# Attention and two MLPs in one kernel: the first eight heads' first queries unsplit, other places for the first MLP's operations, biases in two buffer sets

## The chip, the cores and the metric

The kernel runs on one core of a Trainium2 chip. The metric is the device time of one execution in microseconds (us), the median of several runs. The core has five engines that run side by side and meet at semaphores: TensorE (PE in the rows; its loads of the stationary operand are PEld), VectorE (DVE), ScalarE (ACT), GpSimd (POOL), and SyncE (SP), which issues the DMAs. "Cold" below means TensorE at 1.2 GHz, "warm" at 2.4 GHz.

## What is computed

Four batches of eight heads, 576 positions, head width 64. Per head, with a causal mask and a bias from a running sum, then a soft-max and the product with the values:

```python
scores = scale * np.matmul(q, k.transpose(0, 1, 3, 2))
cum = np.cumsum(np.maximum(s, 0.0), axis=-1)
bias = -(cum[:, :, :, None] - cum[:, :, None, :])
scores = np.where(causal, -1000000000.0, scores + np.minimum(bias, 0.0))
scores = scores - np.max(scores, axis=-1, keepdims=True)
attn = np.exp(scores)
attn = attn / (np.sum(attn, axis=-1, keepdims=True) + 1e-09)
out = np.matmul(attn, v)
```

The heads' outputs, side by side, are 2304 tokens of 512 numbers. They go through a first MLP (512 to 1024, h times its soft-max, a layer norm, 1024 to 512) and a second one (512 to 2048, h * clip(h + 3, 0, 6) / 6, 2048 to 512). All in float32.

## The kernel before

**Arithmetic.** Most products are made of split operands: a float32 tensor x is stored as hi (x rounded to the fp32r type) and lo = x - hi, and TensorE multiplies hi*hi, hi*lo and lo*hi, each in one pass of fp32r. The splits cost ScalarE a copy (hi) and VectorE or GpSimd a subtraction (lo). For q and k, ScalarE makes qk_hi (L1124), GpSimd puts q_lo into the lower half (L610) and makes k_lo (L613), so that one product over 128 rows holds two terms; a second one with k_lo (L722) follows. Probabilities are transposed on TensorE (L736), copied as hi by ScalarE (L1155), and their lo made by VectorE (L953); values are split by GpSimd (L627, L629) and multiplied in two parts (L761), whose halves ScalarE copies (L1163) and VectorE adds (L973).

**Units and items.** A unit is a pair of heads and one of two kinds of queries of it: first queries (0 to 255) or second ones (256 to 575). A batch has four units of the first kind, then four of the second. A unit of the first kind has two items (one a head, with its two tiles of 128 queries), one of the second kind five. So units 0 to 3 are items 0 to 7, units 4 to 7 items 8 to 27, and there are 112 items.

**Slots.** Every engine's program is one loop over slot numbers n, and what it does in slot n is written out by hand (L873 TensorE, L1047 VectorE, L1210 ScalarE, L668 GpSimd, L534 SyncE). In slot n TensorE transposes the probabilities of item n, multiplies the values of a unit that has ended (two slots after its last item began, SUMS_AT), and makes the scores of item n + 2. VectorE takes the bias and the row maximum of item n + 1 (L944) and then splits the probabilities of item n; ScalarE copies those of item n and takes the exponential of item n + 1 (L1132). An engine's instructions run in the order written: one that waits holds up all behind it.

**The first MLP** has 18 tiles of 128 tokens, each with six steps r = 0 to 5, spread evenly over the slots from STARTS[t] to STARTS[t + 1] (L84). Steps 0 to 2: TensorE makes the hidden values (L794), which fill two PSUM banks. Step 3: VectorE takes their maximum (max1, L1009). Step 4: ScalarE takes the exponential (exp1, L1182), VectorE the product with it (solu, L1018). Step 5: ScalarE squares (L1188, written over the hidden values in PSUM), GpSimd makes the reciprocal deviation (L648, L650). In the next tile's step 0 VectorE normalises (L1027), in steps 1 and 2 TensorE transposes (L807), ScalarE copies (L1195), VectorE splits (L1034). Steps 3 to 5 also hold the products with w_out of tile t - 2 (project, L823), whose results VectorE copies (copy_x2, L1040). TensorE may begin the hidden values of tile t + 1 once the squares of tile t are done (L782). A tile's input xs_hi and xs_lo is made by VectorE (L1004) in slot X_AT and by GpSimd (L655) one slot later; X_AT is STARTS[t] - 3, or the slot in which the last unit of these tokens is scaled, if that is later (L184 to L190). That later slot is 10 for tiles 0 and 1, 30 for tile 2, 58 for tile 6, 114 for tile 15.

In slots 3 to 10 ScalarE splits w_in (L1171) in eight parts, VectorE and GpSimd make four lo parts each; from slot 24 on w_out is split (L1176, L997); from slot 120 on GpSimd splits the first weights of the second MLP (L663, L665). SyncE issues nearly all loads in one queue. The bias of a head, its row of the running sum spread over 128 partitions, is loaded from memory into one buffer for each of two heads (L486), after the maximum of the unit that used it before; for unit 0 TensorE spreads it (L869) and ScalarE copies it (L1167).

**The second MLP** follows slot END: 96 rounds of products with 384 columns (L843 to L845) and 512 columns (L860 to L862), where TensorE is busy all the time.

## Time and profile before

| | us |
|---|---|
| median of 3 runs | 921.59 (917.24, 921.59, 922.11) |
| the profiled execution, its own time | 918.19 |
| its span, first to last instruction | 916.4 |
| TensorE busy | 845.5 (92%) |
| VectorE, ScalarE, GpSimd busy | 441.9, 412.8, 296.5 |

The busy time of TensorE is that of pipelined instructions with modelled ends, so "busy" is not "at its peak". The stretch to about 497 us holds attention and the first MLP, the rest the second MLP.

### The profile page before, as it was taken

How to read it: one execution, taken by the hardware profiler on the slowest of the kernel's cores; microseconds unless marked ns; L12 is line 12 of the kernel's file. 1: busy time of each engine (PE TensorE's matmuls, PEld its weight loads, DVE VectorE, ACT ScalarE, POOL GpSimd, SP SyncE). 2: the span in 40 equal slices, each digit the busy share in tenths (PEclk: the TensorE clock that was granted, in tenths of full speed). 3: DMA queues.
4: the chain of work that ended last, by engine and by line, in shares of the span. 5: the costliest groups of instructions: out<-in, count | busy, mean ns of one | idle time of the engine just before them, and what ended most of it. 6: DMA issues, size and time to landing. Idle time of an engine off the chain costs nothing.

```text
span 916.4 us, 13790 instructions
## 1 busy us (share of the span) xinstructions
PE 845.5 (92%) x4916; PEld 750.7 (82%) x4916; DVE 441.9 (48%) x1061; ACT 412.8 (45%) x911; POOL 296.5 (32%) x391
## 2 busy tenths in 40 slices
PE   7778779989899998999898999999999999999997
PEld 5566668888688887888787999989898999999996
DVE  3747767776676767667455232232322232332222
ACT  6745766657566566555223243232322232322222
POOL 7764466455644465453165253000000000000000
PEclk9789879999999999999999999999999999999999
DMA  7536434334434344331402040000000000000000
GB/s 232 176 111 208 119 97 141 96 99 125 124 95 115 91 115 123 108 113 40 137 2 92 1 138 1 35 1 1 35 0 1 35 1 1 35 1 1 35 1 34
DMA packets 39426, 66.84 MB, mean 73 GB/s; under 512 B 4480, under 2 KB 16512, under 8 KB 39360
## 3 DMA queue, kind: packets, MB, share of 16 engines
q1 hardware_dynamic: 39360, 65.97, 23.7%
q8 instruction: 40, 0.66, 0.3%
q14 instruction: 26, 0.21, 0.1%
HBM read 61.16 MB, written 4.79 MB: 72 GB/s over the span
## 4 chain that ended last, share of the span: by engine, by line
PE 69%; DVE 10%; ACT 9%; issue 5%; POOL 4%; DMA 2%; SPq 0%; DVEq 0%; ACTq 0%; POOLq 0%
PE psum L794 9%; PE psum L843 7%; PE psum L845 7%; PE psum L861 7%; PE psum L844 7%; PE psum L862 7%; PE psum L860 7%; PE psum L761 4%; PE psum L823 3%; PE psum L736 3%; ACT prob L1132 3%; ACT p_hi L1155 2%; DVE es L1018 2%; PE psum L807 2%; PE psum L722 2%
## 5 line engine op out<-in xcount | busy, mean ns | idle before, releaser
L1086 DVE SCALAR_TENSOR_TENSOR act<-act,psum 128x384 f32<-128x384 f32 x96 | 53.2, 554 | 286.8 <-ACT act L1240 286.8
L1240 ACT ACTIVATE act<-psum,three 128x384 f32<-128x384 f32 x96 | 55.9, 582 | 285.7 <-PE psum L845 285.7
L843 PE MATMUL psum<-x_hi,w_hi 128*128 128x384 f32 x384 | 129.5, 337 | 0.9 <-DVE x_lo L1044 0.9
L845 PE MATMUL psum<-x_hi,w_lo 128*128 128x384 f32 x384 | 129.5, 337 | 0.0
L844 PE MATMUL psum<-x_lo,w_hi 128*128 128x384 f32 x384 | 129.0, 336 | 0.0
L862 PE MATMUL psum<-w_hi,g_lo 128*128 128x512 f32 x288 | 113.9, 395 | 0.0
L861 PE MATMUL psum<-w_lo,g_hi 128*128 128x512 f32 x288 | 113.7, 395 | 0.0
L860 PE MATMUL psum<-w_hi,g_hi 128*128 128x512 f32 x288 | 112.0, 389 | 0.0
L953 DVE TENSOR_TENSOR p_lo<-psum,p_hi 128x512 fp32r<-128x512 f32 (+2 forms) x128 | 71.9, 572 | 79.5 <-ACT p_hi L1155 79.0
L1155 ACT ACTIVATE p_hi<-psum 128x512 fp32r<-128x512 f32 (+2 forms) x128 | 62.3, 500 | 96.0 <-PE psum L736 63.1
L610 POOL TENSOR_TENSOR qk_hi<-qk_raw,qk_hi 64x256 fp32r<-64x256 f32 (+1 forms) x64 | 57.0, 891 | 125.3 <-ACT qk_hi L1124 124.1
L823 PE MATMUL psum<-lnT_hi,w_out_hi 128*128 128x256 f32 x288 | 83.2, 289 | 9.9 <-DVE xT L1040 9.7
L1132 ACT ACTIVATE prob<-prob,nmax 128x128 f32<-128x128 f32 (+4 forms) x144 | 83.2, 580 | 12.2 <-DVE nmax L944 12.0
L736 PE MATMUL psum<-ident,prob 128*128 128x128 f32 x400 | 67.9, 290 | 20.7 <-ACT prob L1132 17.6
L823 PE MATMUL psum<-lnT_lo,w_out_hi 128*128 128x256 f32 x288 | 82.2, 285 | 0.0
L823 PE MATMUL psum<-lnT_hi,w_out_lo 128*128 128x256 f32 x288 | 82.2, 285 | 0.0
L736 PEld LDWEIGHTS psum<-ident,prob 128*128 128x128 f32 x400 | 49.3, 147 | 33.2 <-ACT prob L1132 28.4
L843 PEld LDWEIGHTS psum<-x_hi,w_hi 128*128 128x128 f32 x384 | 72.1, 188 | 5.3 <-DVE x_lo L1044 1.1
L844 PEld LDWEIGHTS psum<-x_lo,w_hi 128*128 128x128 f32 x384 | 72.1, 188 | 4.0
L722 PE MATMUL psum<-qk_lo,qk_hi 128*128 128x128 f32 (+2 forms) x192 | 73.8, 388 | 0.0
L794 PE MATMUL psum<-w_in_hi,xs_hi 128*128 128x512 f32 x144 | 60.9, 423 | 12.7 <-POOL xs_lo L655 12.7
L613 POOL TENSOR_TENSOR qk_lo<-qk_raw,qk_hi 128x256 fp32r<-128x256 f32 (+1 forms) x64 | 70.9, 1108 | 5.0
(95 smaller groups left out, 1881.6 us busy)
## 6 DMA issues: line engine op xcount, KB each, us to landing
qk_raw<-qk SPq DMA_DIRECT2D x32, 480.0 KB, 3.5
qk_raw<-qk SPq DMA_DIRECT2D x32, 256.0 KB, 2.7
bias<-cum_dram SPq DMA_DIRECT2D x32, 256.0 KB, 3.9
v_raw<-v_rows SPq DMA_DIRECT2D x32, 160.0 KB, 3.1
bias_tail<-cum_dram SPq DMA_DIRECT2D x32, 144.0 KB, 3.8
out<-out_sb SPq DMA_DIRECT2D x6, 768.0 KB, 3.5
w_raw<-w_in SPq DMA_DIRECT2D x16, 256.0 KB, 3.2
w_raw<-w_out SPq DMA_DIRECT2D x16, 256.0 KB, 4.1
```

The lines of the kernel that those rows point to most:

```text
L722: last = pe.matmul(ps, q, qk_lo[p][:, keys], start=False, stop=(part != 0))
L736: last = pe.transpose(dst, prob[:, src:src + P], ident[:, :])
L794: last = pe.matmul(bank(h_bank(t) + half), x, w, start=(n % 12 == 0), stop=(n % 12 == 11))
L823: last = pe.matmul(bank(L_BANK, PJW), w, x, start=(n == 0), stop=(n == 23))
L843: pe.matmul(ps, w2_hi[f][:, cols], xh, start=(c_ == 0), stop=False)
L844: pe.matmul(ps, w2_hi[f][:, cols], xl, start=False, stop=False)
L845: last = pe.matmul(ps, w2_lo[f][:, cols], xh, start=False, stop=(c_ == NC - 1))
L860: pe.matmul(bank(4 + k), gh, w2_hi[f][:, NC * P:], start=(f == 0), stop=False)
L861: pe.matmul(bank(4 + k), gh, w2_lo[f][:, NC * P:], start=False, stop=False)
L862: last = pe.matmul(bank(4 + k), gl, w2_hi[f][:, NC * P:], start=False, stop=(f == NF2 - 1))
L1132: sc.activation(p, p, ACT.Exp, scale=-1.0, bias=nmax[:, u % 2, col:col + 1], accum_out=rsum[:, u % 2, col:col + 1]).then_inc(exp_done, 1)
L1155: sc.activation(hi, ps, ACT.Copy).then_inc(pT_hi_done, 1)
```

## The change

1. **Units 0 to 3** (the first eight heads' first queries, items 0 to 7) are multiplied unsplit. q and k of a pair lie in one float32 tile of 128 partitions, one head in each half (qk_plain), and the scores are float32 products over 64 rows. The bias comes in through TensorE: a product of a one-hot column and the running sum's hi and lo rows (cum_parts) is added into the same PSUM region, and VectorE's maximum reads zeros in the bias's place. VectorE, no longer ScalarE, copies the transposed probabilities, whole; the values are float32 of both heads side by side (v_pair), one product a block; ScalarE copies the sums to their place, and VectorE adds nothing. No split by ScalarE, VectorE or GpSimd is left for these units.
2. The running sum is made first for 256 positions, and whole in VectorE's slot 0.
3. **Biases** lie in one buffer set for each kind of unit, so that a unit of one kind doesn't wait for the set of the other.
4. **Places.** STARTS; w_in is loaded from slot 2 on and split from slot 6 on (before 0 and 3); w_out is loaded in eight parts from slot 15 on (before whole, in slot 18) and split from slot 27 on (before 24).
5. **Order in a slot.** VectorE does max1 (step 3) and solu (step 5, before step 4) right behind the row maxima, ahead of the probabilities. ScalarE does exp1 and the squares behind the probabilities, exponentials and sums (before ahead of them). The squares go to a tile of SBUF, and the next tile's hidden values wait for solu, not for the squares.

```diff
-STARTS = [12, 21, 31, 37, 44, 51, 59, 65, 71, 77, 84, 90, 96, 102, 109, 115, 121, 127, 133]
+STARTS = [13, 25, 33, 39, 45, 54, 60, 66, 72, 78, 84, 90, 96, 103, 110, 116, 122, 129, 135]
-W_IN_FROM, W_OUT_FROM, EARLY_FROM = 3, 24, 120
+W_IN_LOAD = 2
+W_IN_FROM = 6
+W_OUT_LOAD = 15
+W_OUT_FROM = 27
+EARLY_FROM = 120
+PLAIN = 4
+PLAIN_ITEMS = BASE[PLAIN]
...
# SyncE: the first loads
-            load_qk(0, 0)
-            load_qk(0, 1)
-            load_qk(1, 0)
+            for u in range(PAIRS):
+                load_plain(u)
+                load_pair(u)
+            load_qk(PLAIN, 0)
             sp.wait_ge(cum_done, 1)
             sp.dma_start(cum_dram, cum[:, :]).then_inc(cum_stored, 16)
-            load_qk(1, 1)
+            load_qk(PLAIN, 1)
+            load_qk(PLAIN + 1, 0)
             sp.wait_ge(cum_stored, 16)
...
# TensorE: scores of units 0 to 3
+                    if u < PLAIN:
+                        rows = slice(0, P) if e is None else slice(e * DH, (e + 1) * DH)
+                        q = qk_plain[u][rows, q_at:q_at + P]
+                        for lo_, hi_ in [(0, w)] if w <= BANK else [(0, w // 2), (w // 2, w)]:
+                            pe.matmul(psum[:, at + lo_:at + hi_], q, qk_plain[u][rows, QW[c] + lo_:QW[c] + hi_],
+                                      start=True, stop=False)
+                            if n <= 1:
+                                pe.wait_ge(cum_parts_done, n + 1)
+                            h = head_of(u, e)
+                            last = pe.matmul(psum[:, at + lo_:at + hi_], heads[rows, h:h + 1].broadcast_to([DH, P]),
+                                             cum_parts[rows, lo_:hi_], start=False, stop=hi_ <= diag0)
+                            if hi_ > diag0:
+                                mask = mask_tail if e is None else mask_bf
+                                last = pe.matmul(psum[:, at + diag0:at + hi_], ident_bf[:, :], mask[:, 0:hi_ - diag0],
+                                                 start=False, stop=True)
+                        continue
...
# TensorE: their values
+                    if u < PLAIN:
+                        p, v_at = plain_values(u)
+                        last = pe.matmul(psum[:, o_at + q:o_at + width], v_pair[p][:, v_at + j, :, :].rearrange("p a d -> p (a d)"),
+                                         p_plain[:, src:src + width - q], start=(j == 0), stop=(j == blocks - 1))
+                        continue
...
# TensorE: hidden(t)
-                    wait(pe, sq_done, t - 1 if t >= NT - 2 else t)
+                    wait(pe, solu_done, t - 1 if t >= NT - 2 else t)
...
# TensorE: the start
-            pe.wait_ge(cum_done, 1)
-            for e in range(2):
-                pe.matmul(bank(H_BANK + e, CUT), ident[0:NH, e:e + 1].broadcast_to([NH, P]), cum[:, 0:CUT],
-                          start=True, stop=True).then_inc(bias_spread, 1)
             pe.wait_ge(mask_tail_done, 2)
-            pe.wait_ge(zeros_done, 1)
+            pe.wait_ge(heads_done, 2)
...
# VectorE: slot n
                 if 0 <= n + 1 < ITEMS:
                     for tile, e, col in TILES[n + 1]:
                         row_max(n + 1, tile, e, col)
+                if r == 3:
+                    max1(t)
+                if r == 5:
+                    solu(t)
                 if r == 0 and t >= 3:
                     copy_x2(2 * (t - 3) + 1)
-                if 0 <= n < ITEMS:
+                if 0 <= n < PLAIN_ITEMS:
+                    copy_plain(n)
+                    if n == 0:
+                        sum_all()
+                elif 0 <= n < ITEMS:
                     split_probs(n)
+                if n in SCALES_AT:
+                    scale_pair(SCALES_AT[n])
                 if r == 4 and t >= 2:
                     copy_x2(2 * (t - 2))
-                if n in SCALES_AT:
-                    scale_pair(SCALES_AT[n])
...
-                if r == 3:
-                    max1(t)
-                if r == 4:
-                    solu(t)
...
# ScalarE: slot n
-                if r == 4:
-                    exp1(t)
-                if r == 5:
-                    square(t)
-                if 0 <= n < ITEMS:
+                if PLAIN_ITEMS <= n < ITEMS:
                     copy_probs(n)
                 if 0 <= n + 1 < ITEMS:
                     for i, (tile, e, col) in enumerate(TILES[n + 1]):
                         exp_row(n + 1, i, tile, col)
                 for u, e in SUMS_AT.get(n, ()):
-                    copy_corr(u, e)
+                    if u < PLAIN:
+                        copy_sums(u, e)
+                    else:
+                        copy_corr(u, e)
+                if r == 4:
+                    exp1(t)
+                if r == 5:
+                    square(t)
...
-    nc = bacc.Bacc("TRN2", target_bir_lowering=False, num_devices=1)
+    nc = bacc.Bacc("TRN2", target_bir_lowering=False, num_devices=1, dynamic_dma_scratch_size=4096)
```

## Rows read from the trace of the kernel before

**Rows 1.** The page: busy us of each engine, its share of the span, instructions.
```profile
PE 845.5 (92%) x4916; PEld 750.7 (82%) x4916; DVE 441.9 (48%) x1061; ACT 412.8 (45%) x911; POOL 296.5 (32%) x391
```

**Rows 2.** Stretches: busy us (instructions) of PE, PEld, DVE, ACT, POOL; granted clock, DMA share, GB/s.
```profile
51.00:442.00 391.00, 350.79 (x2346) 307.01 (x2347) 265.96 (x697) 240.35 (x557) 203.06 (x283) 0.96 0.37 110
442.00:497.00 55.00, 48.17 (x305) 42.72 (x304) 30.70 (x54) 15.55 (x27) 31.13 (x36) 0.97 0.29 96
```

**Rows 3.** The waits of PE over the span: total us, times, longest.
```profile
PE psum L736 <- ACT prob L1132: 17.6, 23, 2.3
PE psum L794 <- POOL xs_lo L655: 12.7, 4, 3.8
PE psum L823 <- DVE xT L1040: 9.7, 12, 1.5
PE psum L717 <- DVE nmax L944: 5.5, 5, 2.3
```

**Rows 4.** Timeline of PE: start, us, instruction, [idle before <- releaser]; slots 0, 8, 13, and tiles 0, 2.
```profile
9.90 0.90 PE L736 MATMUL psum<-ident,prob 128*128 128x128 f32 x3 [0.30 <-ACT prob L1132]
34.19 0.84 PE L736 MATMUL psum<-ident,prob 128*128 128x128 f32 x3
51.18 0.80 PE L794 MATMUL psum<-w_in_hi,xs_hi 128*128 128x512 f32 x1 [3.77 <-POOL xs_lo L655]
55.86 0.68 PE L736 MATMUL psum<-ident,prob 128*128 128x128 f32 x3
58.16 0.39 PE L794 MATMUL psum<-w_in_lo,xs_hi 128*128 128x512 f32 x1
124.15 0.79 PE L794 MATMUL psum<-w_in_hi,xs_hi 128*128 128x512 f32 x1 [2.95 <-POOL xs_lo L655]
```

**Rows 5.** Timeline of the start: copies of unit 0's spread bias; pace of scores and values.
```profile
6.03 0.38 ACT L1167 ACTIVATE bias<-psum 128x256 f32<-128x256 f32 x1 [0.83 <-PE psum L869]
6.88 0.38 ACT L1167 ACTIVATE bias<-psum 128x256 f32<-128x256 f32 x1 [0.47 <-PE psum L869]
7.39 0.52 PE L717 MATMUL psum<-qk_hi 128*128 128x256 f32 x1
8.62 0.52 PE L717 MATMUL psum<-qk_hi 128*128 128x256 f32 x1
18.25 0.56 PE L761 MATMUL psum<-p_hi,v_sp 128*128 128x256 f32 x1
19.14 0.52 PE L761 MATMUL psum<-p_hi,v_sp 128*128 128x256 f32 x1
```

**Rows 6.** Groups by form, first 34 us: count, busy us, mean ns, idle before.
```profile
L1155 ACT ACTIVATE p_hi<-psum 128x384 fp32r<-128x384 f32 x8 | 3.9, 481 | 1.9 <-PE psum L736 1.9
L1124 ACT ACTIVATE qk_hi<-qk_raw 128x512 fp32r<-128x512 f32 x8 | 4.9, 624 | 2.3 <-DMA qk_raw<-qk 2.3
```

**Rows 7.** Timeline of POOL: the last w_in part before tile 0's xs_lo.
```profile
46.09 1.27 POOL L641 TENSOR_TENSOR w_in_lo<-w_in_raw,w_in_hi 128x512 fp32r<-128x512 f32 x1
```

**Rows 8.** Timeline: tile 10's exp1, what stood behind it, and TensorE's wait.
```profile
347.76 1.12 ACT L1182 ACTIVATE es<-psum,nmax 128x1024 f32<-128x1024 f32 x1 [1.54 <-DVE nmax L1009]
348.86 0.48 ACT L1155 ACTIVATE p_hi<-psum 128x384 fp32r<-128x384 f32 x1
350.41 0.35 PE L823 MATMUL psum<-lnT_hi,w_out_hi 128*128 128x256 f32 x1 [1.42 <-DVE xT L1040]
```

**Rows 9.** The squares and exp1, every one: duration ns min/median/max, first and last start.
```profile
L1188 ACT ACTIVATE psum<-es,neg_mu x18: 1101/1119/1122, 77.1 to 492.6; 128x1024 f32<-128x1024 f32 x18
L1182 ACT ACTIVATE es<-psum,nmax x18: 1093/1117/1120, 70.7 to 489.4; 128x1024 f32<-128x1024 f32 x18
```

**Rows 10.** ScalarE in slot 28: w_out's split.
```profile
111.55 0.71 ACT L1176 ACTIVATE w_out_hi<-w_out_raw,g_sb 128x512 fp32r<-128x512 f32 x1
```

**Rows 11.** Timeline of DVE, after attention: max1 of tiles 15 and 16.
```profile
459.96 1.22 DVE L1009 TENSOR_REDUCE nmax<-psum 128x1 f32<-128x1024 f32 x1 [0.52 <-PE psum L794]
473.21 1.23 DVE L1009 TENSOR_REDUCE nmax<-psum 128x1 f32<-128x1024 f32 x1 [0.53 <-PE psum L794]
```

More of the change, by code:

```diff
@@ L140, in buffer_of, with los, seconds, plain_values @@
 def buffer_of(load):
-    return 3 + load if load < OWN else (load - OWN) % 3
+    return load % 3
 def loads_of_buffer(load):
-    return 1 if load < OWN else (load - OWN) // 3 + 1
+    return load // 3 + 1
+def los(n):
+    return LOS_BEFORE[n] - LOS_BEFORE[PLAIN_ITEMS]
+def seconds(u):
+    return sum(not k for k in FIRST_KIND[PLAIN:u + 1])
+def plain_values(u):
+    if FIRST_KIND[u]:
+        return u // 2 % 2, u % 2 * 2
+    return u % 2, 0
 SUMS_AT = {}
@@ L157 @@
 SPLIT_AT = {}
-for _u in range(UNITS):
+for _u in range(PLAIN, UNITS):
     for _e in range(2):
-        if load_of(_u, _e) < OWN:
-            _n = max(-3, load_of(_u, _e) - 5)
-        elif _u == PAIRS:
+        if _u == PLAIN:
             _n = BASE[_u] - 5 + _e
@@ L190, with build @@
 SPLIT_X_AT = {n + 1: t for n, t in X_AT.items()}
-def build(nc, qk0, qk1, v_rows, s, w_in, w_out, g_ln, w2_in, w2_out, cum_dram, out):
+def build(nc, qk0, qk1, plain0, plain1, v_rows, v_pairs, s, w_in, w_out, g_ln, w2_in, w2_out, cum_dram, out):
     with ExitStack() as ctx:
@@ L221, in build @@
         three = sb(ctx, "three", [P, 1])
+        half_heads = sb(ctx, "half_heads", [P, DH])
+        heads = sb(ctx, "heads", [P, NH], F32R)
+        zeros = sb(ctx, "zeros", [P, CUT])
         first = ExitStack()
@@ L257, in build @@
         with ExitStack() as own:
-            for p in range(3, 3 + OWN):
-                qk_buffer(own, p, QW[1] + KN[1])
+            qk_plain = [sb(own, f"qk_plain{u}", [P, QW[kind(u)] + KN[kind(u)]]) for u in range(PLAIN)]
         w_out_hi = sb(first, "w_out_hi", [P, NF1, DM], F32R)
@@ L270, in build @@
         es = sb(first, "es", [P, F1])
+        squares = sb(first, "squares", [P, F1])
         xs_hi = sb(first, "xs_hi", [P, NC, P], F32R)
@@ L456, in bias_loads @@
         def bias_loads(u):
-            return len(units_of_half(u)) - (1 if half_of(u) == half_of(0) else 0)
+            return sum(bias_place(m) == bias_place(u) for m in range(PLAIN, u + 1))
         def tokens(u):
@@ L475, in load_qk @@
                     else:
-                        sp.wait_ge(tail_half_ready, sum(not k for k in FIRST_KIND[:u_ + 1]))
+                        sp.wait_ge(tail_half_ready, seconds(u_))
                 w = QW[c] + KN[c]
@@ L549, in _ @@
                             load_bias_tail(u)
-                for u in range(2, UNITS):
+                for u in range(PLAIN, UNITS):
                     for e in range(2):
@@ L1289, with pairs @@
     values = np.concatenate([v, np.zeros((NH, NQ * P - SEQ, DH), np.float32)], axis=1)
+    values = values.reshape(NH, NQ, P, DH).transpose(0, 2, 1, 3)
+    def pairs(x):
+        return x[:HEADS].reshape(PAIRS, 2 * DH, x.shape[2])
+    first = np.concatenate([qT[:, :, :CUT], kT[:, :, :CUT]], axis=2)
+    second = np.concatenate([qT[:, :, CUT:cut], tails, kT], axis=2)
     def twice(x):
@@ L1295 @@
     arrays = {
-        "qk0": twice(np.concatenate([qT[:, :, :CUT], kT[:, :, :CUT]], axis=2)),
-        "qk1": twice(np.concatenate([qT[:, :, CUT:cut], tails, kT], axis=2)),
-        "v_rows": values.reshape(NH, NQ, P, DH).transpose(0, 2, 1, 3),
+        "qk0": twice(first),
+        "qk1": twice(second),
+        "plain0": pairs(first),
+        "plain1": pairs(second),
+        "v_rows": values,
+        "v_pairs": values[:HEADS].reshape(PAIRS, 2, P, NQ, DH).transpose(0, 2, 3, 1, 4),
         "s": s.reshape(NH, SEQ),
```

226 lines of the change are left out of this document (146 added, 80 removed).

## The prediction

> **What bounds the kernel now.** First the page: TensorE is busy 845.5 of 916.4 us [rows 1], so it is idle for 70.9 us, and no change can gain more than that plus what TensorE loses to its low clock. Next the stretches: of 391 us from 51 to 442 (attention and first MLP together) TensorE is busy 350.79, at a mean granted clock of 0.96; from 442 to 497, 48.17 of 55 [rows 2]. What comes behind is untouched by the change. So 40.2 us of idle time lie in the middle stretch and 6.8 in the one behind it; of the other 24 us the larger part lies ahead of 51 us. Then the waits: TensorE stood 17.6 us for exponentials, 12.7 for xs_lo (four times), 9.7 for copy_x2, 5.5 for row maxima [rows 3]. Last the timeline: slot 0 begins at 9.90 us, slot 8 at 34.19, tile 0's hidden values at 51.18 behind 3.77 us of waiting, slot 13 at 55.86 [rows 4]. That is 3.0 us a slot in slots 0 to 7, which hold little for TensorE. TensorE is the bound in the middle, the hand-over between engines is it at the start.
>
> A measurement of this kernel can tell about 0.5% (4.6 us) from no change. The sum is made against the profiled execution's 918.19 us (span 916.4 and 1.8 around it); the median of the runs shown is 3.4 us higher.
>
> **Part 1, units 0 to 3 unsplit.** *TensorE's added work.* An item of a head had 128 + 128 + 128 and 256 + 128 + 256 = 1024 columns of scores; it now has four passes of 128 and of 256, one pass of the bias for each, and two masks of 128: 2176. Values of a head: 2 parts x (256 + 128) = 768 before, 4 passes x 384 = 1536 now. Over eight heads that is 8 x (1152 + 768) = 15,360 columns more, 12.8 us at 1.2 GHz or 6.4 us at 2.4. That float32 costs four passes is in the trace: the two 256-column float32 products that spread unit 0's bias were handed over at 6.03 and 6.88 [rows 5], 0.85 us apart, which is 4 x 256 / 1.2 GHz.
>
> *Its pace.* Scores of one head took 8.62 - 7.39 = 1.23 us [rows 5] for 1024 columns, 0.853 us at 1.2 GHz; the other 0.38 us are six weight loads, 0.063 each. The new head has eight instruction pairs (a float32 product counts twice, as the spread bias's x4 for two products did): 1.81 + 0.50 = 2.3 us cold, and about 1.15 warm. Values took 19.14 - 18.25 = 0.89 us a head [rows 5] cold; new 1.28 + 0.17 = 1.45 cold, 0.75 warm. Three transposes take 0.75 us cold (the 0.90 of [rows 4] less what overlaps with the next product), and I take 0.45 warm. A slot of TensorE is then 3.05 us cold without values and 4.5 with them (from slot 3 on), and 1.6 and 2.35 warm.
>
> *What goes.* ScalarE loses eight copies of 0.481 us and eight splits of 0.624 [rows 6]: 1.1 us a slot in which it was busiest. Its exponentials and sums remain, and the copy goes to VectorE, where it stands in place of a subtraction of like length: nothing there. GpSimd loses eight q/k splits and eight value splits, all in slots that did not end on GpSimd: nothing by itself. The start loses the wait for the whole running sum, for the copies of the spread bias and for the first q/k split. The 256-position sum and its hi and lo cost VectorE four more short instructions on 32 partitions, about what the shorter sum saves (an estimate); GpSimd's two new additions for `heads` lie beside the first DMAs' flight. I take slot 0 at about 9.0 us, 0.9 earlier.
>
> *The clock.* The q/k, bias and value products leave no idle time on a cold TensorE, while before every slot had a wait. Before, a dense run of hidden values began cold at 51.18 (0.80 us for the first of 512 columns), and at 58.16 one took 0.39 [rows 4], so dense work did bring the high clock. I take the high clock from about 12 us on: slot 0 3.05 us, slots 1 and 2 2.0 each (the 3.0 of before less the 1.1 that ScalarE is freed of), five slots of 2.4: slot 8 at 9.0 + 3.05 + 4.0 + 12.0 = 28.1, 6.1 us earlier than 34.19 [rows 4]. Bounds: low clock in slots 0 to 3, slot 8 at 9.0 + 9.15 + 4.5 + 9.6 = 32.3 (1.9 gained); high clock from slot 0, 27.0 (7.2 gained).
>
> **Part 2, slots 8 to 13.** Before, 21.67 us from slot 8 to slot 13 [rows 4], with 3.77 us for xs_lo and eight hidden values at the low clock (8 x 512 / 1.2 GHz = 3.4). GpSimd made w_in's lo parts ahead of xs_lo, 1.27 us each [rows 7], three of them in slots 8 to 10. Now w_in's parts are three slots later, behind xs_lo, and tile 0 starts one slot later: the last two parts (2.5 us) and a slot of 2.8 are 5.3 us of new slack against a wait of 3.77, so it goes. ScalarE's w_in splits stay in these slots, so I take 2.8 us a slot, not less ((21.67 - 3.77 - 3.4) / 5 = 2.9 before). Five of them and eight warm hidden values of 0.23: 15.9 us to the same place, 5.8 gained. Bounds: 2 (only half the wait goes) and 8.
>
> **Part 3, the other three waits for xs_lo.** Tiles 2, 6 and 15 began in the slot right after X_AT, where GpSimd makes xs_lo: 12.7 - 3.77 = 8.9 us [rows 3, 4]. Each now begins at least one slot later (33, 60, 116). Tile 2's wait of 2.95 lies among first-kind slots, where ScalarE is late next; I take 2 of it, and 8.0 in all. Two low-clock stretches of 3.4 us each follow the last two; half of that, and a little for tile 2's, gives 3. Bounds 4 and 13 together.
>
> **Part 4, the orders.** Tile 10's exp1 waited 1.54 us for max1 at the head of ScalarE's slot and ran 1.12; the copy of probabilities came behind it at 348.86, copy_x2 behind that, and TensorE waited 1.42 us [rows 8]. Now exp1 stands behind the copy. The waits for exponentials, copy_x2 and maxima are 17.6 + 9.7 + 5.5 = 32.8 us [rows 3], a quarter of it at the start and in the tail by my reading of the stretches: 24 are left. Part of them has another cause (w_out's splits among them), and where one goes the next engine is late soon after: 10 us, between 2 and 24. copy_x2 now stands behind scale_pair in the few slots that have both; I take nothing, as it is much less than what exp1 gives back. The earlier release of hidden values (solu instead of squares) is worth nothing in the middle, as TensorE's slot is full then.
>
> The squares now go to SBUF. The row: squares into PSUM take 1119 ns, exp1 of the same size into SBUF 1117 [rows 9]; I take nothing. The Trainium skill, ScalarE: Activation LUTs, section "Step-by-step: what each stage is for", says that ScalarE writes PSUM with less delay than SBUF. By that the squares would be slower now; the trace does not bear it out, and as step 5's square is followed by 5 us or more of other work the sum would not move by a few hundredths each.
>
> **Part 5, the rest.** Biases in two sets: VectorE is shown waiting for no bias. SyncE's waits for a maximum at a change of kind held q/k loads behind them, though; 0 to 3 us, I take 0.5. w_out's splits move from slots 24 to 31 to slots 27 to 34: three more of 0.71 us [rows 10] in slots where ScalarE is the bound, -2.1. In SyncE's queue the split w_out load adds seven issues in slots with time to spare. Behind attention: tile 14 has one step more to go, which moves work and adds none; a tile there takes 473.21 - 459.96 = 13.25 us [rows 11], six slots, nearly all of it TensorE's. GpSimd has seven of the second MLP's early splits ahead of tile 17's input instead of five, but does one of them in idle time first: up to 2 us, I take 1.
>
> **The sum.** 6.1 + 5.8 + 8.0 + 3 + 10 + 0.5 - 2.1 - 1 = 30.3 us; 918.2 - 30.3 = 888 us.
>
> **Rivals.**
> *A, the start alone.* What is freed in the middle is taken by the next late engine, since TensorE's slots there are 90% full. For it: part 4's waits are 40 of less than 1 us each on average [rows 3]. Against: the waits for xs_lo are 2.4 to 3.8 us each and have one cause. 918.2 - 11.9 = 906 us. Chance 0.20.
> *B, the order was the bound.* All 24 us of part 4's waits went through VectorE's and ScalarE's late slot heads, and the other parts are worth 24 too: 918.2 - 48 = 870 us. For it: 40.2 us are idle in the middle [rows 2]. Chance 0.12.
> *C, TensorE's own work is the bound (slower).* The idle time removed was cover for pipelined work, and the 15,360 columns are added where TensorE stays at 1.2 GHz through slots 3 to 7: slot 8 comes at 9.0 + 9.15 + 22.5 = 40.7, 6.5 us later than before, and all behind follows, its waits given back in full. 918.2 + 6.5 to 12.8: 925 to 931 us. It decides if the clock stays low beyond slot 5. For it: values still took 0.89 us a head at 18.25 before, the cold pace [rows 5], though TensorE was busy by then for most of each slot. Against: every one of slots 0 to 7 had a hand-over in it then. Chance 0.08.
> *D, no change.* The clock rises late (1.9 gained at the start), and w_out's splits in first-kind slots and the crowd on GpSimd in slots 9 to 11 take back the rest: about 917 us. Chance 0.06.
>
> My forecast has 0.54. The range leaves out C and D (0.14) and the deep end of B: 868 (B) to 911 (A with part 1 between its term and its lower bound). Faster by over 0.5%: forecast, A and B, 0.86; within 0.5%: 0.06; slower: 0.08.
>
> **What would show it.** Right: slot 8's transposes before 30 us, values of units 1 to 3 with the high clock, no wait for xs_lo over 1 us, exp1's wait for max1 gone, fewer waits for copy_x2, slot 13 near 44 us, the middle stretch's idle time near 20 us. Wrong: float32 products of 256 columns that take 0.85 us beyond 22 us (C); the same 40 us of idle time under new names (A); ScalarE's slots of 4 us and more in items 28 to 35, with TensorE waiting for exponentials there (D).

## The result, and the profile after

| | before | changed |
|---|---|---|
| median of the runs shown | 921.84 us (917.24 to 922.11) | 888.1 us (884.16 to 892.73) |
| profiled execution | 918.19 us, span 916.4 | 891.85 us, span 890.1 |

The ratio is 0.9647, 95% interval 0.9578 to 0.9716: 33.7 us less by the medians. The forecast was 888. Its sum does not stand as it was made, though: one term of it gave nothing, one gave somewhat less and two gave more than they were booked at, and that these errors cancel is luck.

The page of the changed kernel, its head and part 1 (the engines' busy time), beside [rows 1]:

```profile
span 890.1 us, 13740 instructions
PE 848.6 (95%) x4928; PEld 753.2 (85%) x4928; DVE 436.1 (49%) x1059; ACT 405.4 (46%) x893; POOL 282.1 (32%) x361
```

TensorE is idle for 41.5 us instead of 70.9, and ScalarE and GpSimd have lost the splits of eight heads. Next the stretches, as in [rows 2], and behind them three short ones that are read further down (start and end, length, then busy time and count of PE, PEld, DVE, ACT, POOL, then granted clock, DMA share, GB/s):

```profile
0.00:51.00 51.00, 43.22 (x174) 31.14 (x174) 26.60 (x85) 26.98 (x72) 17.95 (x31) 0.94 0.51 160
51.00:442.00 391.00, 368.97 (x2506) 326.00 (x2507) 277.05 (x726) 249.67 (x572) 220.99 (x300) 0.98 0.40 119
442.00:497.00 55.00, 48.44 (x298) 44.91 (x297) 23.38 (x39) 15.28 (x27) 23.93 (x24) 0.94 0.13 39
4.04:21.00 16.96, 16.96 (x56) 11.62 (x57) 8.09 (x32) 4.91 (x20) 0.40 (x1) 1.00 0.67 222
19.30:31.00 11.70, 11.70 (x41) 9.08 (x41) 4.21 (x18) 5.72 (x16) 5.14 (x5) 1.00 0.59 186
465.00:472.00 7.00, 6.29 (x20) 6.30 (x21) 2.20 (x4) 0.64 (x2) 0.55 (x1) 0.51 0.03 12
```

In the middle stretch 18.2 of 40.2 us of idle time are gone. TensorE's waits over the whole span, beside [rows 3] (who waited, for whom: us, times, longest):

```profile
PE psum L834 <- ACT prob L1270: 9.3, 14, 1.7
PE psum L834 <- DVE p_lo L1086: 7.0, 5, 3.6
PE psum L929 <- DVE xT L1173: 5.3, 11, 0.6
PE psum L796 <- DMA qk_plain<-plain: 4.0, 1, 4.0
PE psum L949 <- DVE x_lo L1177: 2.6, 1, 2.6
PE psum L900 <- POOL xs_lo L723: 0.8, 1, 0.8
```

The four waits for xs_lo (12.7 us) have become one of 0.8, those for exponentials have halved (17.6 to 9.3), and those for copy_x2 went from 9.7 to 5.3. One kind of wait grew: that for the lo parts of the probabilities, which VectorE now makes behind max1 and solu, is 7.0 us. Before, it was:

```profile
PE psum L736 <- DVE p_lo L953: 2.5, 3, 1.1
```

So the middle went as argued in the main. The start did not. TensorE's timeline there, beside [rows 4, 5] (start, duration, engine, line, operation, output and inputs, shapes, count, idle time before it and what ended it):

```profile
4.04 0.77 PE L796 MATMUL psum<-qk_plain 64*128 64x128 f32 x2 [4.04 <-DMA qk_plain<-plain]
8.01 1.22 PE L796 MATMUL psum<-qk_plain 64*128 64x256 f32 x2
9.45 0.85 PE L834 MATMUL psum<-ident,prob 128*128 128x128 f32 x3
19.27 0.85 PE L834 MATMUL psum<-ident,prob 128*128 128x128 f32 x3
19.91 1.91 PE L863 MATMUL psum<-p_plain,v_pair 128*128 128x256 f32 x5
33.32 0.50 PE L834 MATMUL psum<-ident,prob 128*128 128x128 f32 x3
37.29 0.49 PE L834 MATMUL psum<-ident,prob 128*128 128x128 f32 x3
465.70 0.69 PE L949 MATMUL psum<-x_hi,w_hi 128*128 128x384 f32 x1 [2.63 <-DVE x_lo L1177]
```

Slot 0's transposes begin at 9.45, slot 3's at 19.27: 3.27 us a slot. Three transposes take 0.85 us there and 0.50 at 33.32. (A float32 product of q and k, as the one of 256 columns at 8.01, counts as two instructions in the rows.)
### The profile page after: what moved, and what is told of

The parts are those of the page before. It is cut to its first block, busy times and chain, and to the rows that moved or that the text cites. A ratio compares the mean times of both kernels' runs of the same rounds, so it can differ in the third digit from the quotient of the medians.

```text
span 890.1 us, 13740 instructions
## 1 busy us (share of the span) xinstructions
PE 848.6 (95%) x4928; PEld 753.2 (85%) x4928; DVE 436.1 (49%) x1059; ACT 405.4 (46%) x893; POOL 282.1 (32%) x361
## 4 chain that ended last, share of the span: by engine, by line
PE 83%; ACT 6%; DVE 5%; issue 3%; POOL 2%; DMA 0%; ACTq 0%; DVEq 0%; SPq 0%; POOLq 0%
PE psum L900 9%; PE psum L929 9%; PE psum L949 8%; PE psum L951 8%; PE psum L950 8%; PE psum L967 8%; PE psum L968 8%; PE psum L966 7%; PE psum L867 5%; PE psum L834 4%; PE psum L818 2%; PE psum L813 2%; ACT prob L1270 2%; PE psum L796 2%; PE psum L913 2%
## 5 line engine op out<-in xcount | busy, mean ns | idle before, releaser
L1383 ACT ACTIVATE act<-psum,three 128x384 f32<-128x384 f32 x96 | 55.9, 582 | 288.5 <-PE psum L951 288.5
L1293 ACT ACTIVATE p_hi<-psum 128x384 fp32r<-128x384 f32 (+1 forms) x120 | 58.6, 503 | 102.5 <-PE psum L834 67.6
L1086 DVE TENSOR_TENSOR p_lo<-psum,p_hi 128x384 fp32r<-128x384 f32 (+1 forms) x120 | 67.2, 571 | 54.7 <-ACT p_hi L1293 54.5
L679 POOL TENSOR_TENSOR qk_hi<-qk_raw,qk_hi 64x384 fp32r<-64x384 f32 (+1 forms) x56 | 50.4, 900 | 106.0 <-ACT qk_hi L1262 104.4
L951 PEld LDWEIGHTS psum<-x_hi,w_lo 128*128 128x128 f32 x384 | 72.9, 190 | 0.0
L834 PEld LDWEIGHTS psum<-ident,prob 128*128 128x128 f32 x400 | 49.0, 147 | 26.5 <-ACT prob L1270 17.7
L682 POOL TENSOR_TENSOR qk_lo<-qk_raw,qk_hi 128x576 fp32r<-128x576 f32 (+1 forms) x56 | 67.7, 1209 | 4.4
L818 PE MATMUL psum<-qk_lo,qk_hi 128*128 128x288 f32 (+4 forms) x176 | 65.3, 376 | 0.0
```

What stands on the lines that cost most here:

```text
L682: pool.tensor_tensor(qk_lo[p][:, k_cols], qk_raw[p][:, k_cols], qk_hi[p][:, k_cols].bitcast(F32), ALU.subtract).then_inc(k_lo_done, 1)
L818: last = pe.matmul(ps, q, qk_lo[p][:, keys], start=False, stop=(part != 0))
L834: last = pe.transpose(dst, prob[:, src:src + P], ident[:, :])
L951: last = pe.matmul(ps, w2_lo[f][:, cols], xh, start=False, stop=(c_ == NC - 1))
```

## Where the profiled execution's time went

Beginnings of the same work in both traces, in us:

| place | before | changed | gained |
|---|---|---|---|
| slot 8's transposes | 34.2 | 37.3 | -3.1 |
| slot 13's transposes | 55.9 | 51.0 | 4.9 |
| max1 of tile 6 | 248.5 | 231.9 | 16.6 |
| max1 of tile 10 | 346.5 | 321.2 | 25.3 |
| max1 of tile 14 | 442.1 | 414.0 | 28.1 |
| max1 of tile 17 (last) | 488.2 | 457.3 | 30.9 |
| second MLP's first product | 494.9 | 465.7 | 29.2 |
| the end (whole time) | 918.2 | 891.9 | 26.3 |

The row of slot 13 flatters the change: before, eight hidden values of tile 0 lie ahead of these transposes (slot 12), now they follow them (slot 13) and take from 54.02 to 56.59. At the same work, 51.04 + 2.57 = 53.6 stands against 55.9, a lead of 2.3 us. (Where STARTS has moved a tile by a slot, as tiles 6 and 14, the rows of max1 err a little the other way.) From there to tile 10 come 23 us more. Two of the old waits for xs_lo lie in that stretch, so it is not the order's alone; experiments 6, 7 and 10 part them. At the end 4.6 us are given back. VectorE's timeline of the changed kernel shows where:

```profile
457.33 1.21 DVE L1142 TENSOR_REDUCE nmax<-psum 128x1 f32<-128x1024 f32 x1
460.22 1.37 DVE L1177 TENSOR_TENSOR x_lo<-xT,x_hi 128x384 fp32r<-128x384 f32 x1 [0.39 <-ACT x_hi L1347]
461.89 1.28 DVE L1151 SCALAR_TENSOR_TENSOR es<-psum,rden,es 128x1024 f32<-128x1024 f32 x1
465.09 0.56 DVE L1177 TENSOR_TENSOR x_lo<-xT,x_hi 128x384 fp32r<-128x384 f32 x1 [1.72 <-ACT x_hi L1347]
```

The last tile's solu now stands in step 5, behind an x_lo of step 4, and the chain of the last tile ends later by it: TensorE waits 2.63 us for the last x_lo, and then runs at the low level (0.51 in the stretch from 465 to 472 us). From there to the end of the span this execution takes 424.4 us, 2.9 more than before. The wait belongs to the new order: it is 2.6 us in order_only, both_edits and split_all too, and 0.9 in starts_only and order_undone. The low level behind it comes in some executions only. In experiment 9, the same kernel, the wait is 2.6 us as well, the clock does not fall, and the rest takes 421.5 us, as before:

```profile
442.00:497.00 55.00, 49.08 (x314) 45.41 (x313) 23.89 (x38) 16.42 (x29) 21.52 (x20) 1.00 0.15 48
```

## Experiments

The kernel before ran beside each group of kernels, with medians of 920.04 us (the first four), 920.97 (the next four) and 920.72 (the last four). An interval is the ratio's to it, at 95%.

**1. The old way of multiplying, with the new order and places (split_all).** Before, plus:

```diff
-STARTS = [12, 21, 31, ...
+STARTS = [13, 25, 33, ...
-W_IN_FROM, W_OUT_FROM, EARLY_FROM = 3, 24, 120
+W_IN_FROM, W_OUT_FROM, EARLY_FROM = 6, 27, 120
# orders of VectorE and ScalarE as in the change, squares to SBUF
-                    wait(pe, sq_done, t - 1 if t >= NT - 2 else t)
+                    wait(pe, solu_done, t - 1 if t >= NT - 2 else t)
```

One bias set, w_out loaded whole in slot 18, all units split.

> The kernel before with the new STARTS, the new slots of the w_in and w_out splits, the new order in a slot and the squares in SBUF; all units split, one bias set, w_out loaded whole. Theory 1 (the unsplit units gave little, because TensorE stayed at 1.2 GHz until 31.5 us and slot 8 came 3 us later than before; what they gave back is GpSimd's and ScalarE's time in slots 8 to 13): 889 to 893 us, at most 5 above the changed kernel. Rival (the prediction's parts 1 and 2, the start alone is worth 11.9 us): about 900 us. If the time lies below the changed kernel's, the unsplit units cost something.

Measured: 885.15 us (884.48 to 886.44), 0.9622 [0.9608, 0.9636]. TensorE's timeline at slot 8:

```profile
31.14 0.52 PE L737 MATMUL psum<-ident,prob 128*128 128x128 f32 x3
```

Its stretch in the middle:

```profile
51.00:442.00 391.00, 369.88 (x2535) 327.33 (x2535) 280.52 (x731) 250.41 (x573) 221.21 (x303) 0.99 0.39 118
```

That is below the range of theory 1 and below the changed kernel. The whole gain is there without the unsplit products, and slot 8 comes at 31.14, 6 us ahead of the changed kernel's first profile and 2.3 ahead of its second one (experiment 9). The middle is the same to 1 us. Part 1 of the change, together with the two bias sets and the split w_out load, gives nothing.

**2. The order undone (order_undone).** The changed kernel with max1, solu, exp1, the squares and copy_x2 at their old places in the slots; the squares still go to SBUF.

```diff
 # VectorE
-                if r == 3:
-                    max1(t)
-                if r == 5:
-                    solu(t)
...
+                if r == 3:
+                    max1(t)
+                if r == 4:
+                    solu(t)
 # ScalarE
+                if r == 4:
+                    exp1(t)
+                if r == 5:
+                    square(t)
                 if PLAIN_ITEMS <= n < ITEMS:
                     copy_probs(n)
...
-                if r == 4:
-                    exp1(t)
-                if r == 5:
-                    square(t)
```

> The changed kernel with max1, solu, exp1, squares and copy_x2 at their old places in a slot (squares still go to SBUF). Theory 1 (part 4 of the prediction, the order is worth 10 us): 896 to 902 us, waits for copy_x2 and exponentials back to 9 and 12 us. Rival A (what the order frees is taken by the next late engine): 888 to 891 us. Rival B (the order is most of the gain): over 908 us.

Measured: 904.83 us (904.6 to 909.74), 0.9843 [0.9819, 0.9867]: 18 us slower than the changed kernel run again (experiment 9), more than theory 1 had and less than rival B. TensorE's waits:

```profile
PE psum L834 <- ACT prob L1270: 18.1, 21, 2.5
PE psum L929 <- DVE xT L1173: 9.1, 13, 1.4
```

Exponentials and copy_x2 are back at the values of [rows 3] (17.6 and 9.7), so it is the order that halves them. Which of its moves does how much (max1 and solu, exp1 and the squares, the hidden values that wait for solu) was not tried one by one.

**3. The old start slots (starts_undone).** The changed kernel with `STARTS = [12, 21, 31, ...]` of before and nothing else.

> The changed kernel with the old STARTS alone. Theory 1 (the waits for xs_lo come from tiles that begin in the slot after X_AT): the waits of tiles 2, 6 and 15 for xs_lo are back, 2.4 to 3.5 us each, with low-clock stretches behind them: 897 to 901 us. Rival (other slack in the slots takes them up, now that GpSimd has less to do at the start): 888 to 891 us.

Measured: 912.44 us (908.63 to 913.18), 0.9904 [0.9886, 0.9923]. Its waits:

```profile
PE psum L900 <- POOL xs_lo L723: 10.8, 5, 3.6
PE psum L929 <- DVE w_out_lo L1130: 5.7, 1, 5.7
```

The time is over both ranges. xs_lo is back, and the later w_out slots are now too late for a tile that starts earlier. So this run charges the start slots with a wait that they never had before; experiment 5 takes it away.

**4. The last solu earlier (last_solu).** The changed kernel with tile 17's solu in step 4:

```diff
-                if r == 5:
+                if r == 5 and t < NT - 1:
                     solu(t)
...
+                if r == 4 and t == NT - 1:
+                    solu(t)
```

> The changed kernel with the last tile's solu in step 4 again, as before the change (all other tiles in step 5). In the changed kernel the second MLP began 8.4 us after the last max1, 6.7 before the change, and TensorE waited 2.63 us for x_lo and then ran at 1.2 GHz for 6.8 us. Theory 1 (the last solu behind a split of x2 delays the squares and the last x_hi): the wait falls to 1 us; 1.7 us gained, and up to 3.4 more if the low clock goes with it: 883 to 886 us. Rival (the second MLP's start hangs on something else, such as copy_x2): no difference, 888 us.

Measured: 888.43 us (883.44 to 889.27), 0.9644 [0.9621, 0.9667]. VectorE's timeline:

```profile
459.12 1.21 DVE L1142 TENSOR_REDUCE nmax<-psum 128x1 f32<-128x1024 f32 x1
461.99 1.29 DVE L1151 SCALAR_TENSOR_TENSOR es<-psum,rden,es 128x1024 f32<-128x1024 f32 x1
```

TensorE's wait for the last x_lo:

```profile
PE psum L949 <- DVE x_lo L1177: 0.9, 1, 0.9
```

The place itself did what it should: solu follows max1 by 2.9 us instead of 4.6, and TensorE waits 0.9 us. The second MLP starts at the high level, but so it did in experiment 9 without this edit. In this execution the clock had risen only at 37.5 us, by its transposes' durations. The median is the rival's: it shows no gain, and could hardly show one of 1.7 us, with the start varying by more than that.

**5. Start slots and w slots undone (places_undone).** As 3, with `W_IN_LOAD = 0`, `W_IN_FROM = 3` and `W_OUT_FROM = 24` as well.

> The changed kernel with the old STARTS and the old slots of the w_in loads and splits and of the w_out splits. With the old STARTS alone it took 912.4 us, but TensorE then waited 5.7 us for w_out's lo part, whose split had stayed three slots later. Theory 1 (STARTS is worth the three waits for xs_lo and what follows, and 6 us of the 24 were w_out's): 903 to 907 us. Rival (w_in's splits of slots 8 to 10, ahead of xs_lo, are back and tile 0 waits too): 907 to 912 us.

Measured: 908.66 us (906.99 to 913.06), 0.9879 [0.9849, 0.9909]. The time is in the rival's range. The wait for w_out_lo is gone, xs_lo stays, five times now, tile 0's among them:

```profile
PE psum L900 <- POOL xs_lo L723: 12.4, 5, 3.5
```

908.66 - 886.9 (experiment 9) = 22 us are what all the places are worth once the order is the new one.

**6. and 7. One edit alone in the kernel before.** starts_only is before with the new STARTS; order_only is before with the new order, the squares in SBUF and the wait for solu. (In these, and in the kernels 1, 10 and 11 that are built on before, the transposes' wait names the last slot that used the same bank, as the old formula holds for the old first step only; SyncE's scratch is as in the change.)

```diff
-                before = n - 2 if n <= FIRST_STEP else n - 1
+                before = max([m for m in range(n) if turn(m) == turn(n)], default=-1)
```

> The kernel before with the new STARTS alone (and the smaller DMA scratch). Theory 1 (the two edits overlap little: order_undone and starts_undone lose 17 and 18 to 24 us of 35): 900 to 904 us, no wait for xs_lo over 1 us. Rival (each edit alone gives little, as the other hand-over then is late): over 910 us.

> The kernel before with the new order in a slot, squares in SBUF and hidden values that wait for solu, and nothing else. Theory 1: 903 to 907 us, the waits for copy_x2 at 5 us and those for xs_lo unchanged at 12 us. Rival (both needed): over 910 us.

Measured: starts_only 907.69 us (906.02 to 908.96), 0.9855 [0.9827, 0.9882]; order_only 906.64 us (904.92 to 908.5), 0.9848 [0.9823, 0.9874]. TensorE's waits of starts_only:

```profile
PE psum L736 <- ACT prob L1132: 19.3, 23, 2.3
PE psum L823 <- DVE xT L1040: 9.1, 13, 1.5
PE psum L794 <- POOL xs_lo L655: 2.3, 2, 1.2
```

and of order_only:

```profile
PE psum L795 <- POOL xs_lo L656: 12.9, 4, 3.8
PE psum L737 <- ACT prob L1133: 9.0, 15, 1.3
PE psum L824 <- DVE xT L1041: 4.8, 9, 0.6
```

Each edit removes its own waits and leaves the other's nearly as they were: 13.3 us by the start slots (theory 1 had 17 to 21), 14.3 by the order, as theory 1 had. In starts_only w_in is split in its old slots, and tile 0 still waits for no xs_lo: the one slot by which it begins later is enough.

**8. More rows in the early products (rows128).** The changed kernel, but q times k of units 0 to 3 runs over all 128 partitions. This changes the computation: both heads of such a pair get the sum of the two heads' scores. Columns and instructions are the same.

```diff
-                        q = qk_plain[u][rows, q_at:q_at + P]
+                        q = qk_plain[u][:, q_at:q_at + P]
...
-                            pe.matmul(psum[:, at + lo_:at + hi_], q, qk_plain[u][rows, QW[c] + lo_:QW[c] + hi_],
+                            pe.matmul(psum[:, at + lo_:at + hi_], q, qk_plain[u][:, QW[c] + lo_:QW[c] + hi_],
```

> The changed kernel with the products of q and k of units 0 to 3 over all 128 rows of the pair's tile instead of the 64 of one head: the scores are then the sum of both heads' (this part of the computation is changed), at the same count of columns and passes. The changed kernel's TensorE had no idle time from 4.0 to 31.5 us and still ran at 1.2 GHz; kernels with the same first slots rose at 21.5, 22.3, 31.5 and 37.5 us. Theory 1 (products over half the rows do not bring the high clock): it rises by 15 us, slot 8 comes before 30 us, 882 to 885 us with a small spread. Rival (the rows do not matter; float32 passes or the chance of the moment do): it rises anywhere from 21 to 38 us, slot 8 at 33 to 39 us, median near 888.

Measured: 886.72 us (885.38 to 889.06), 0.963 [0.9603, 0.9658]; the clock rose at 24.2 us and slot 8 came at 34.70:

```profile
34.70 0.49 PE L834 MATMUL psum<-ident,prob 128*128 128x128 f32 x3
```

That is 7 us ahead of the first profile's rise, but experiment 9 rises at 22.9 with 64 rows. The signs are the rival's. The idea that half-filled rows hold the clock down finds no support. (The product that adds the bias still has 64 rows here.)

**9. The changed kernel again (changed_again).** No edit.

> The changed kernel once more, on the chip of the next three. Theory 1 (its start runs at 1.2 GHz until 21 to 38 us, by the moment, and that spreads it over 884 to 893 us): the profile again shows the rise somewhere in that range, and slot 8 follows it; the median is 885 to 890, at or above split_all's 885.2. Rival (the unsplit units gain a little): under 885 us.

Measured: 886.9 us (884.08 to 888.65), 0.9637 [0.9615, 0.966]; its profiled execution took 884.08 us, and slot 8 came here:

```profile
33.45 0.49 PE L834 MATMUL psum<-ident,prob 128*128 128x128 f32 x3
```

The same program had its clock risen at 31.5 us in one execution and at 22.9 in the other, slot 8 differs by 3.8 us, the second MLP's first product by 5.0 (465.7 against 460.7), and the whole times by 7.8. So of these two executions' difference half arises at the start, and most of the rest in the low stretch behind the last wait. The time and the rise are as theory 1 had them.

**10. Start slots and order together (both_edits).** Before with the edits of 6 and 7, w_in and w_out at their old places.

> The kernel before with the new STARTS and the new order, but the old slots of the w_in and w_out splits; units split. starts_only gained 13.3 us, order_only 14.3, split_all 35.8: 8.2 more than the two together. Theory 1 (the slots of w_in's and w_out's splits are those 8 us): 891 to 895 us. Rival (the two edits help each other, since each removes the wait that the other leaves): 885 to 888 us.

Measured: 888.43 us (887.14 to 890.31), 0.966 [0.9639, 0.968]. That is 32.3 us, where the two alone give 27.6: 4.7 more, nearly the rival's range. Part 1 of the pages, first of starts_only (span 906.2 us), then of order_only (906.7) and both_edits (885.4), shows what kind of time it is; [rows 1] has that of before (916.4):

```profile
PE 846.5 (93%) x4916; PEld 753.6 (83%) x4916; DVE 437.7 (48%) x1061; ACT 413.3 (46%) x911; POOL 295.6 (33%) x391
PE 850.7 (94%) x4916; PEld 758.3 (84%) x4916; DVE 438.5 (48%) x1061; ACT 412.7 (46%) x911; POOL 296.6 (33%) x391
PE 840.6 (95%) x4916; PEld 749.2 (85%) x4916; DVE 438.1 (49%) x1061; ACT 413.5 (47%) x911; POOL 296.9 (34%) x391
```

TensorE's idle time falls from 70.9 us to 59.7 with the start slots, to 56.0 with the order and to 44.8 with both: 11.2 and 14.9 alone, 26.1 together, so it adds up. The surplus is in the busy time. The same 4916 instructions take 846.5 and 850.7 us alone (845.5 before), and 840.6 together. That is the share of the low level: the mean clock from 51 to 442 us is 0.97, 0.95 and 0.98. (In these four executions the surplus is 11 us, by the medians 4.7. Why the clock is low less often with both is not shown.)

The new slots of the w_in and w_out splits are the rest of split_all: 888.43 - 885.15 = 3.3 us. The traces have them at the start, where only w_in's splits lie: slot 8 comes at 34.2 to 34.4 us in the four split kernels with w_in in its old slots (before, starts_only, order_only, both_edits), and at 31.1 and 32.1 in split_all and split_best, where ScalarE has no w_in part to split in slots 3 to 5.

**11. Best of both (split_best).** split_all with the edit of 4.

> split_all with the last tile's solu in step 4. last_solu's profile showed the wait for x_lo at 0.9 instead of 2.6 us and the second MLP's first rounds at 2.4 GHz, while its median (888.4) hid it in the spread of its start. split_all has a small spread. Theory 1: 882 to 884 us, faster than both kernels. Rival (nothing gained): 885 us.

Measured: 882.87 us (882.45 to 883.46), 0.9597 [0.9579, 0.9615]. As theory 1 had it, it beats both kernels: 37.9 us under before, 4.0 under the changed kernel beside it. Against split_all, its slowest run (883.46) lies below the other's fastest (884.48). The stretch behind attention, against 49.08 busy and a clock of 0.97 in split_all's:

```profile
442.00:497.00 55.00, 50.78 (x325) 47.10 (x326) 24.00 (x41) 16.43 (x29) 22.56 (x21) 1.00 0.16 52
```

**12. A warmed TensorE (warm_up).** The changed kernel with eleven bf16 products of 512 columns ahead of the first scores; nothing reads them.

```diff
             pe.wait_ge(consts_done, 4)
+            for _ in range(11):
+                pe.matmul(bank(H_BANK), ident_bf[:, :], ident_bf[:, 0:1].broadcast_to([P, BANK]), start=True, stop=True)
```

> The changed kernel with 11 products of 512 columns (bfloat16, 128 rows, into an idle PSUM bank, results unused) ahead of the first scores: 4.7 us at 1.2 GHz, from about 2.8 us on, which delay the first scores by some 3.5 us. Theory 1 (the unsplit start is bound by TensorE at 1.2 GHz, and the scores do not bring the high clock): the clock rises by 12 us, slots 0 to 2 take 2.0 us or less instead of 3.3, slot 8 comes at 28 to 30 us: 880 to 883 us. Rival (the clock falls back or does not rise, or ScalarE and VectorE bound the slots): slot 8 at 37 us or later, 889 to 893 us.

Measured: 884.13 us (881.38 to 890.45), 0.9623 [0.959, 0.9656]. TensorE's timeline:

```profile
2.96 4.34 PE L973 MATMUL psum<-ident_bf 128*128 128x512 bf16 x11 [2.96 <-POOL three L669]
7.87 0.70 PE L796 MATMUL psum<-qk_plain 64*128 64x256 f32 x2
10.38 0.55 PE L834 MATMUL psum<-ident,prob 128*128 128x128 f32 x3
12.31 0.50 PE L834 MATMUL psum<-ident,prob 128*128 128x128 f32 x3
28.51 0.49 PE L834 MATMUL psum<-ident,prob 128*128 128x128 f32 x3
```

Now a float32 product of 256 columns takes 0.70 us instead of 1.22, slots 0 and 1 are 1.9 us apart, and slot 8 comes at 28.51. From slot 0 to slot 8 that is 18.1 us; the prediction's price for a high clock from slot 0 on was 27.0 - 9.0 = 18.0. The median lies 1 us above theory 1's range. At slot 28 the lead over experiment 9 is 3.8 us (90.0 against 93.8), at the end 2.8 by the medians, which six runs from 881 to 890 us do not hold apart.

## Why the prediction came out right, step by step

**Part 1 failed, in its step on the clock.** "I take the high clock from about 12 us on" was the step. The runs of the changed kernel show the rise at 31.5 and 22.9 us, with TensorE busy without a gap up to 21 us. With a late rise slot 8 lies at 33.5 to 37.3 against 34.19, so where 6.1 us were booked, +0.7 to -3.1 were seen, outside the bounds of 1.9 to 7.2. The prices of the slots were near: 3.05 us for a cold slot without values (3.27 measured), and 18.0 from slot 0 to slot 8 with a high clock (18.1 in warm_up). What the +0.7 to -3.1 leave out is that split kernels gain there too: w_in's later slots bring their slot 8 from 34.4 to 31.1 and 32.1 (experiment 10), for which the prediction had no term. Against those the changed kernel's slot 8 comes 1.4 to 6.2 us late. With units unsplit the same later slots bring nothing there: slot 8 comes at 37.2 in places_undone and at 37.3 in the first profile, with the clock's rise at 31.4 and 31.5. Over the whole kernel the medians put the unsplit way 1.8 us behind the split one (886.9 to 885.15, whose intervals overlap), and 5.6 behind it with the last solu moved (888.43 to 882.87, whose intervals do not). Both pairs were run beside different runs of before and include the bias sets and the w_out load; the sign is likely, the size is not settled. Rival C had the right mechanism, extra columns where TensorE stays slow, but its condition (low beyond slot 5) was met in one profile only, experiment 4's, with slot 8 at 39.3 (the rival had 40.7), and there too the waits behind it stayed away.

**Part 2 held.** From slot 8 to slot 13 it took 21.67 us before, and takes 51.04 - 37.29 = 13.75 now (13.2 in experiment 9). The forecast of 15.9 counts tile 0's eight hidden values in, which now come behind slot 13's transposes and take 2.6 us (2.3 in experiment 9). With them it is 16.3 and 15.5: 5.4 and 6.2 gained, 5.8 forecast. The cause is the one given, the wait of 3.77 us for xs_lo is gone; but of the two reasons for it the slot by which tile 0 begins later was enough (experiment 6), and w_in's later parts were not needed for it.

**Part 3 held in kind and nearly in size.** Parts 2 and 3 with the clock's share were 5.8 + 8 + 3 = 16.8 us; starts_only gives 13.3. Moving w_out's splits had been booked as a loss of 2.1, in "slots where ScalarE is the bound". All w slots together gain 3.3, and by slot 8's times that is w_in's, in split kernels. Whether w_out's splits cost their 2.1 there was not tried.

**Part 4 was mis-sized.** 10 us stood in the sum, of 2 to 24. The order is worth 14.3 us alone, 18 by undoing it. "Where one goes the next engine is late soon after" took off too much: it did happen, with the wait for the probabilities' lo parts that went from 2.5 to 7.0 us, but waits for exponentials and copy_x2 fell by 8.3 and 4.4 us, and TensorE's idle time by 14.9 with the order alone. The clock is not the order's: alone it leaves the middle at 0.95 (before 0.96 [rows 2]), and only with the new start slots it is 0.98. The mechanism shows at tile 10. ScalarE's timeline there has exp1 at the end of its slot, with no wait, as max1 ran from 321.22 to 322.44:

```profile
321.45 0.49 ACT L1293 ACTIVATE p_hi<-psum 128x384 fp32r<-128x384 f32 x1 [1.25 <-PE psum L834]
326.70 1.10 ACT L1325 ACTIVATE es<-psum,nmax 128x1024 f32<-128x1024 f32 x1
```

In [rows 8] it stood 1.54 us at the head of the slot with the copy of probabilities behind it. Waits for exp1's maximum were 26.5 us over the kernel before, and are 7.9 now. ScalarE's group of exp1 before (busy, mean ns of one, idle time ahead of it and its releaser):

```profile
L1182 ACT ACTIVATE es<-psum,nmax 128x1024 f32<-128x1024 f32 x18 | 20.1, 1114 | 26.5 <-DVE nmax L1009 26.5
```

The same group of the changed kernel:

```profile
L1325 ACT ACTIVATE es<-psum,nmax 128x1024 f32<-128x1024 f32 x18 | 19.9, 1108 | 8.0 <-DVE nmax L1142 7.9
```

Every square of the changed kernel (ns min/median/max, first and last start):

```profile
L1331 ACT ACTIVATE squares<-es,neg_mu x18: 1137/1151/1155, 85.4 to 463.4; 128x1024 f32<-128x1024 f32 x18
```

The squares into SBUF take 1151 ns, into PSUM they took 1119 [rows 9]. The rule weighed in the prediction (the Trainium skill, ScalarE: Activation LUTs, section "Step-by-step: what each stage is for") has the right direction for them: 0.03 us each, 0.6 us of ScalarE in all. That this did not move the sum is argued, not shown; no kernel had the new order with squares in PSUM.

**Part 5.** The loss behind attention was expected on GpSimd, 1 us. It came on VectorE, by the last solu: 1.7 us of waiting more than before, and in the first profile 2.9 us of low clock behind it. The bias sets were not tried apart.

**The sum.** Put together from the runs: 13.3 + 14.3 + 4.7 + 3.3 = 35.6, less 1.8 for the rest of the change, 33.8 us. (It is a chain of differences from before to the changed kernel, so its total comes out by construction; what it tells is the shares.) Forecast were 30.3. The number came out by luck: part 1, 6 us too high and more, was made up by the order and its interplay with the starts, some 9 too low if the 4.7 of interplay are all put with the order. (Term by term against the forecast: -7.9 for part 1, +9.0 for the order, -3.5 for the starts, +5.4 for the w slots; +0.5 is left for biases and the work behind attention, which these runs don't part from part 1.) Of the signs named in advance, four came (xs_lo, exp1's wait but for three of 2.5 to 2.9 us behind attention, copy_x2, the middle's idle time of 22 against 20), and two did not: slot 8 before 30 us, and slot 13 near 44 us (51.0 and 46.6, even without the hidden values that the 44 counts in). Values of units 1 to 3 ran at the high clock in experiment 9; in the first profile unit 1's did not.

**Left open.** Why the clock stays low so long at the start. It is not idle time (none in 17 us), and not plainly the rows of the q/k products (24.2 against 22.9 us). Whether it is the float32 products themselves was not tried on its own. The six profiles of kernels that split all units rise at 22.1 to 26.8 us, the seven with unsplit units and no extra products at 21.5 to 37.5: the late rises (31.4, 31.5, 37.5) are all among the unsplit, but four of those seven are as early as the others.

## What to carry over

Where two engines hand work over in every slot, put the long operation that nobody waits for at once behind the short one that the bound engine waits for, and start a block one slot after its inputs are ready: two such edits removed different waits and were worth more together (32.3 us) than apart (27.6). A TensorE without idle time was not a fast TensorE at this kernel's start; before adding columns there in exchange for another engine's time, cost them at 1.2 GHz, and there read durations, not the clock column. When two traces are compared at a slot, ask whether the same work lies ahead of it. And a new order that is right for all tiles can be wrong for the last one, whose chain nothing covers: look at it by itself.

## What the runs showed of the hardware

- In the 13 profiled executions without the extra products (before, the changed kernel and eleven others) TensorE's clock rose between 21.5 and 37.5 us, before's at 22.1 us with idle time of 0.2 to 1.0 us ahead of the transposes of slots 0 to 3, the changed kernel's at 31.5 and 22.9 with none from 4.04 to 21 us in the first. With eleven dense bf16 products ahead it was up by 6.6 us.
- After its rise it fell again for stretches in the slots that follow (45.2 to 55.4 us in the changed kernel's first profile), and in that profile once more behind a wait of 2.63 us (465 to 472). In the second profile of the same kernel it did not fall behind a wait of 2.60 us at the same place.
- The start slots and the order each took idle time from TensorE (11.2 and 14.9 us), and with the order alone its busy time grew by 5.2 us for the same instructions, at a clock of 0.95 instead of 0.96 in the middle.
- Some kernels spread more than others: the runs of split_all lie within 2.0 us, those of the changed kernel within 8.6, of warm_up within 9.1. In warm_up the two slowest runs (889.9 and 890.5 us) have a mean granted clock of 0.976 and 0.974, the other four 0.981 to 0.984.
